# Outputs of one recurrence unit and scores of the next share one hook of an even step, half of the scores in the gate's bank

## The chip, the cores and the metric

The kernel runs on one core of a Trainium2 chip. The metric is the device time of one execution in microseconds (us); the time of a version is the median of its runs. Engines are called as in the profile: PE is TensorE, PEld its weight loads, DVE is VectorE, ACT is ScalarE, POOL is GpSimd, SP is SyncE, which issues most of the transfers.

## The reference

Three layers run one after the other: a linear-attention recurrence with decay (4 batches, 8 heads, 768 steps, head size 48), a dense gated layer (384 to 1536 and back, on 3072 tokens), and a mixture of 8 experts of which each token takes one.

```python
for t in range(S):                       # recurrence, per batch and head
    cur = einsum('bhd,bhe->bhde', u * k[t], v[t])
    y[t] = einsum('bhd,bhde->bhe', r[t], state + cur)
    state = w * state + einsum('bhd,bhe->bhde', k[t], v[t])
...
g = x @ w_gate                           # dense layer
x2 = (g * sigmoid(g) * (x @ w_val)) @ w_out
...
e_idx = argmax(x2 @ w_gate2)             # expert layer, one expert per token
out[mask] = gate_w * eom * (relu(x2[mask] @ w1[e]) @ w2[e])
```

## The kernel before

**Units.** The recurrence is cut into 6 chunks of 128 steps. A unit is one chunk of one batch (all 8 heads), so there are 24 units, `Unit(c, b)` with number `u.i = 4*c + b`. A unit has three pieces of work on PE: `scores(u)` (keys by receptances, L1615 and L1619), `outputs(u)` (the old state by receptances at L1646, then the masked scores by values at L1661 and L1672) and `state_terms(u)` (keys by values, L1689). Around them POOL scales keys and receptances by powers of the decay into `KW`, `RW` and `KH`; DVE sums the own terms (`sum_own`, L1107), masks the scores into `AM` (`mask_scores`, L1101, one instruction for each half of the scores, which stand in two PSUM banks), adds the state (`add_state`, L1132), the diagonals (`add_diagonals`, L1114) and the outputs into `X1` (`add_output`, L1124); ACT makes the diagonals (L793) and copies half of the outputs (`copy_output`). All matrices are single precision; the large products are split into high and low parts, three matmuls for one.

**Blocks and steps.** The dense layer runs in 6 blocks n of 512 tokens (one chunk of all 4 batches), each of 12 steps f, one for each 128 of the 1536 hidden values. In a step PE computes the gate (`up(GATE_PS, ...)`, 9 matmuls of 512 columns, L1734) and the value (`up(VALUE_PS, ...)`, 9 more), then, if there is one, a hook of recurrence work, then `down(n, f-1)` (9 matmuls, L1782 to L1784), the output product of the step before. The gate stands in bank 0, the value in bank 1, the outputs of the block in banks 2 to 4. ACT applies Silu to the gate (L868) and copies the high part (`AH`); DVE multiplies by the value (`PP`, L1325) and makes the low part (`AL`, L1328). Block n carries the 4 units of chunk n+1 in hooks of the steps 0 to 7; block 5 carries none. The order on every engine is written out by hand, and semaphores join them.

**Order of the hooks.** At an even step f PE does `state_terms` of the unit before and `scores` of unit f/2; at the odd step after it `outputs` of the same unit. The scores and the outputs of a unit share banks 5 and 6, so `scores(u)` waits until DVE has added the outputs of the unit before (`y_added`). Step 0 of a block from the second on has `turn` and `route_logits` (transposes and router logits of the block before) ahead of the hook, and the steps 9 and 10 have two small pieces of the router.

**First block.** Here the dense weights are also split. `STG` receives a piece of weights for two steps (six such pieces), ACT copies the high part (`WH`, three instructions), and DVE subtracts to get the low part (`WL`, `dense_lows`, L1142, three instructions of a third each, behind its hook work of an even step). PE waits for all three thirds of a piece (`dense_low`) before the gate of that piece's first step, and so ahead of steps 1, 2, 4, 6, 8 and 10:

```python
if first and (f == 1 or (f and f % 2 == 0)):
    pe.wait_ge(dense_low, 3 * (f // 2) + 3)
need(pe, silu_ready, q)
up(GATE_PS, 0, f, n).then_inc(gate_ready, 1)
need(pe, value_free, q)
...
up(VALUE_PS, 1, f, n).then_inc(value_ready, 1)
```

After the dense layer come 19 tiles of the expert layer, whose code the change does not touch.

Of the kernel before, what the change touches and what calls it, by code (L numbers as in the profile page):

```python
# [118 lines left out]
def rwkv_moe_moe(nc, unit_rk, unit_v, consts, w_dense, w_route, w1, w2, out):  # L119
# [89 lines left out]
    RW = place(a, "RW", [PR, PAIRS * P])  # L209
    KH = place(a, "KH", [P, PAIRS * PR])  # L210
# [80 lines left out]
    class Unit:  # L291
# [4 lines left out]
        def __init__(self, c, b):  # L296
# [21 lines left out]
            self.out = slice(b * P, b * P + P)  # L318

# [9 lines left out]
    def unit_before(u):  # L329
        return Unit(u.c, u.b - 1) if u.b else Unit(u.c - 1, BATCH - 1)  # L330
# [10 lines left out]
    with ctx:  # L341
# [139 lines left out]
        def _(sp):  # L481
# [8 lines left out]
            def load_two_ahead(u):  # L490
# [143 lines left out]
        def _(pool):  # L634
# [32 lines left out]
            def scale_r(u):  # L667
# [4 lines left out]
                else:  # L672
                    pool.wait_ge(y_ready, u.behind)
# [87 lines left out]
        def _(act):  # L761
# [18 lines left out]
            def first_state(b):  # L780
                u = Unit(0, b)
                act.wait_ge(u_ready, b // 2 * 2 + 2)
                for s in range(PAIRS):
                    last = nc.scalar.activation(ST[:, b, s, :], u.u[0:PR, s * VW:s * VW + VW], ACT.Copy, scale=WPOW[:, s, 7:8])
# [70 lines left out]
            def dense_block(n):  # L855
                first = isinstance(n, int) and n == 0
                last = isinstance(n, int) and n == CH - 1
                units = [] if last else units_of_block(n)
# [5 lines left out]
                for f in range(FT):  # L864
# [19 lines left out]
                    if f // 2 < len(units):  # L884
                        if f % 2 == 0:
                            diagonals(units[f // 2])
                        else:
                            copy_output(units[f // 2], n)
# [110 lines left out]
            with act.Fori(1, CH - 1) as n:  # L999
                dense_block(n)  # L1000
            dense_block(CH - 1)
# [27 lines left out]
        def _(dve):  # L1029
# [97 lines left out]
            def add_state(u):  # L1127
                dve.wait_ge(u_ready, u.i + 1)
                dve.wait_ge(state_ready, u.i - BATCH + 1)
                for s in range(PAIRS):  # L1130
                    used = Head(s).used
                    last = stt(out=ST[:, u.b, s, used], in0=ST[:, u.b, s, used], scalar=WPOW[:, s, 7:8],  # L1132
                               in1=u.u[0:PR, s * VW + used.start:s * VW + used.stop], op0=ALU.mult, op1=ALU.add)
# [175 lines left out]
            def dense_block(n):  # L1309
                first = isinstance(n, int) and n == 0  # L1310
                last = isinstance(n, int) and n == CH - 1
                units = [] if last else units_of_block(n)
# [3 lines left out]
                for f in range(FT):  # L1316
# [37 lines left out]
                    if f // 2 < len(units):  # L1354
                        u = units[f // 2]
                        if f % 2 == 0:
                            sum_own(u)
# [214 lines left out]
        def _(pe):  # L1572
# [288 lines left out]
            def dense_block(n):  # L1861
# [3 lines left out]
                for f in range(FT):  # L1865
# [6 lines left out]
                    if f == 1 and not first:  # L1872
                        pe.wait_ge(logits_copied, n)
# [187 lines left out]
```

## Time and profile before

| what | before |
|---|---|
| median of 3 runs | 836.19 us (835.34 to 836.27) |
| profiled execution, its time | 837.2 us |
| profiled execution, its span | 835.4 us |
| PE busy | 818.8 us, 98% |
| DVE, ACT, POOL busy | 485.8, 368.5, 201.2 us |
| granted PE clock | 0.999 of full speed |

PE is busy nearly the whole span, but its matmuls are pipelined and overlap in the record: a matmul of 512 columns is shown as 0.39 us long and the next one starts 0.23 us after it. So the busy share says little, and the distance from one start to the next is what is read here. In a timeline row the first number is the start in us from the span's start, the second the length of the group of equal instructions; a small matmul in full precision is recorded twice, so 16 of them stand as x32.

### The profile page before, as it was taken

How to read it: one execution, taken by the hardware profiler on the slowest of the kernel's cores; microseconds unless marked ns; L12 is line 12 of the kernel's file. 1: busy time of each engine (PE TensorE's matmuls, PEld its weight loads, DVE VectorE, ACT ScalarE, POOL GpSimd, SP SyncE). 2: the span in 40 equal slices, each digit the busy share in tenths (PEclk: the TensorE clock that was granted, in tenths of full speed). 3: DMA queues.
4: the chain of work that ended last, by engine and by line, in shares of the span. 5: the costliest groups of instructions: out<-in, count | busy, mean ns of one | idle time of the engine just before them, and what ended most of it. 6: DMA issues, size and time to landing. Idle time of an engine off the chain costs nothing.

```text
span 835.4 us, 19888 instructions
## 1 busy us (share of the span) xinstructions
PE 818.8 (98%) x7813; PEld 718.3 (86%) x7813; DVE 485.8 (58%) x1004; ACT 368.5 (44%) x705; POOL 201.2 (24%) x159
## 2 busy tenths in 40 slices
PE   7999999999999999999999999999999999999996
PEld 4777788888888888888888888899999999999996
DVE  7767635335543454435343453469968877897771
ACT  3644334223332143324332322456566776687661
POOL 3434204432354043502420210004021111111010
PEclk9999999999999999999999999999999999999999
DMA  8455203111221022302200116057997668766700
GB/s 336 159 170 170 70 4 119 62 60 40 88 96 61 10 90 85 98 1 97 87 1 2 39 39 260 6 223 230 336 389 261 244 252 294 294 251 242 285 18 19
DMA packets 24146, 116.72 MB, mean 140 GB/s; under 512 B 3372, under 2 KB 9824, under 8 KB 18448
## 3 DMA queue, kind: packets, MB, share of 16 engines
q1 hardware_dynamic: 19984, 101.16, 34.1%
q0 software_dynamic: 3520, 9.87, 3.1%
q10 hardware_dynamic: 576, 4.72, 1.6%
q8 instruction: 52, 0.85, 0.4%
q14 instruction: 14, 0.11, 0.0%
HBM read 102.64 MB, written 14.16 MB: 140 GB/s over the span
## 4 chain that ended last, share of the span: by engine, by line
PE 86%; DVE 7%; ACT 1%; issue 1%; DMA 1%; POOLq 0%; DVEq 0%; ACTq 0%
PE bank L1734 33%; PE bank L1782 6%; PE bank L1784 5%; PE bank L1783 5%; PE bank L1857 5%; PE bank L1855 5%; PE bank L1856 4%; PE bank L1816 3%; PE bank L1821 3%; PE bank L1822 3%; PE bank L1820 3%; DVE WL L1142 2%; PE bank L1661 1%; PE bank L1817 1%; PE bank L1615 1%
## 5 line engine op out<-in xcount | busy, mean ns | idle before, releaser
L1734 PE MATMUL bank<-X1H,WH 128*128 128x512 f32 x432 | 169.1, 392 | 2.6 <-DVE WL L1142 2.6
L1734 PE MATMUL bank<-X1L,WH 128*128 128x512 f32 x432 | 168.0, 390 | 0.2 <-DVE X1L L1148 0.2
L1734 PE MATMUL bank<-X1H,WL 128*128 128x512 f32 x432 | 168.0, 390 | 0.0
L1325 DVE TENSOR_TENSOR PP<-SG,bank 128x512 f32<-128x512 f32 (+1 forms) x78 | 49.8, 645 | 200.4 <-PE bank L1734 184.6
L763 ACT ACTIVATE AH<-PP 128x512 fp32r<-128x512 f32 (+1 forms) x78 | 46.0, 597 | 167.7 <-DVE PP L1325 167.7
L868 ACT ACTIVATE SG<-bank 128x512 f32<-128x512 f32 x72 | 43.0, 597 | 138.5 <-PE bank L1734 138.5
L1734 PEld LDWEIGHTS bank<-X1H,WH 128*128 128x128 f32 x432 | 81.0, 188 | 21.3 <-DVE WL L1142 4.3
L1734 PEld LDWEIGHTS bank<-X1H,WL 128*128 128x128 f32 x432 | 81.0, 188 | 17.3 <-DVE WL L1142 0.3
L1734 PEld LDWEIGHTS bank<-X1L,WH 128*128 128x128 f32 x432 | 81.1, 188 | 16.9 <-DVE X1L L1148 0.6
L1782 PE MATMUL bank<-AH,WH 128*128 128x512 f32 (+1 forms) x234 | 92.1, 394 | 0.0
L746 POOL DMA_INDIRECT out<-YO,IDX x31 | 38.7, 1248 | 218.1 <-ACT YO L962 208.9
L1784 PE MATMUL bank<-AH,WL 128*128 128x512 f32 (+1 forms) x234 | 87.7, 375 | 0.0
L1783 PE MATMUL bank<-AL,WH 128*128 128x512 f32 (+1 forms) x234 | 87.5, 374 | 0.0
L1328 DVE TENSOR_TENSOR AL<-PP,AH 128x512 fp32r<-128x512 f32 (+1 forms) x78 | 54.0, 699 | 51.2 <-ACT AH L763 51.2
L725 POOL DMA_INDIRECT store<-RC,POSI x24 | 26.0, 1084 | 199.0 <-DVE POSI L1240 171.4
L1782 PEld LDWEIGHTS bank<-AH,WH 128*128 128x128 f32 x234 | 44.0, 188 | 10.9
L793 ACT ACTIVATE DIAG<-CST,OWN_SUM 128x64 f32<-128x64 f32 x160 | 40.5, 336 | 29.2 <-DVE OWN_SUM L1107 27.7
L1822 PE MATMUL bank<-XH,W1L_ODD 128*128 128x256 f32 x189 | 52.2, 276 | 0.0
L1820 PE MATMUL bank<-XH,W1H_ODD 128*128 128x256 f32 x189 | 52.2, 276 | 0.0
L1821 PE MATMUL bank<-XL,W1H_ODD 128*128 128x256 f32 x189 | 52.2, 276 | 0.0
L1784 PEld LDWEIGHTS bank<-AH,WL 128*128 128x128 f32 x234 | 44.1, 188 | 8.1
L1783 PEld LDWEIGHTS bank<-AL,WH 128*128 128x128 f32 x234 | 44.2, 189 | 6.6
(238 smaller groups left out, 1825.4 us busy)
## 6 DMA issues: line engine op xcount, KB each, us to landing
W_EVEN<-w SPq DMA_DIRECT2D x20, 1536.0 KB, 8.5
W_ODD<-w SPq DMA_DIRECT2D x18, 1536.0 KB, 8.4
RK_IN<-unit_rk SPq DMA_DIRECT2D x19, 736.0 KB, 5.4
V_IN<-unit_v SPq DMA_DIRECT2D x20, 480.0 KB, 3.7
STG<-w_dense ACTq DMA_DIRECT2D x4, 1152.0 KB, 5.2
XG_ODD<-store SPq DMA_DIRECT2D x9, 394.0 KB, 8.6
store<-PAD SPq DMA_DIRECT2D x8, 394.0 KB, 5.2
STG<-w_dense SPq DMA_DIRECT2D x2, 1152.0 KB, 9.3
```

The source lines that it names most:

```text
L763: return nc.scalar.activation(out_, in_, ACT.Copy)
L868: nc.scalar.activation(SG[:, :], GATE_PS[:, :], ACT.Silu).then_inc(silu_ready, 1)
L1325: return tt(PP[:, part], SG[:, part], VALUE_PS[:, part], ALU.mult)
L1328: return tt(AL[:, par, part], PP[:, part], AH[:, par, part], ALU.subtract)
L1734: last = mm(bank_[:, :], lhs[:, f, m, k * P:k * P + P], rhs[:, k, :], start=(x == 0), stop=(x == len(terms) - 1))
L1782: mm(O_PS[m][:, t], WH[:, f, 2, w], AH[:, par, t], start=(f == 0), stop=False)
L1783: mm(O_PS[m][:, t], WH[:, f, 2, w], AL[:, par, t], start=False, stop=False)
L1784: last = mm(O_PS[m][:, t], WL[:, f, 2, w], AH[:, par, t], start=False, stop=(f == FT - 1 and x == 1))
L1820: mm(to, wh[:, w[k]], XH[:, k, :], start=(k == 0), stop=False)
L1821: mm(to, wh[:, w[k]], XL[:, k, :], start=False, stop=False)
L1822: last = mm(to, wl[:, w[k]], XH[:, k, :], start=False, stop=(k == KT - 1))
L1855: mm(YO_PS[half][:, 0:DM], HH[:, f, tk], wh[:, w], start=(f == 0), stop=False)
```

## The change

`outputs` of a unit move from an odd step into the even step after it, between `state_terms` of that unit and `scores` of the next one. So a hook of steps 2, 4, 6 and 8 has state terms and outputs of the unit that ends and scores of the unit that begins; the odd steps and step 0 (but for the first block's) have no hook. The scores get banks of their own: one half in bank 0, which is the gate's, the other in bank 7. The state terms go to the free columns of banks 5 and 6. `RW` gets a second buffer. In the first block the wait for the low weights is cut up, and the lows of the second piece are spread over two steps.

```diff
-                self.kw, self.rw, self.kh, self.am = KW, RW, KH, AM_PARTS
-                self.scores = self.y = bank[5], bank[6]
-                self.u = bank[7][:, PAIRS * VW:2 * PAIRS * VW]
+                self.kw, self.rw, self.kh, self.am = KW, (RW, RW_ODD)[self.odd], KH, AM_PARTS
+                self.scores = bank[0], bank[7]
+                self.y = bank[5], bank[6]
...
+    def unit_begun(n, f):
+
+        final = isinstance(n, int) and n >= CH - 2
+        if f in (2, 4, 6) and not (final and n == CH - 1):
+            return units_of_block(n)[f // 2]
+        if f == 0 and isinstance(n, int) and n == 0:
+            return units_of_block(n)[0]
+        if f == 8 and not final:
+            return units_of_block(n + 1)[0]
+        return None
+
+    def unit_ended(n, f):
+
+        if f in (2, 4, 6, 8) and not (isinstance(n, int) and n == CH - 1):
+            return units_of_block(n)[f // 2 - 1]
+        return None
...
                 def v_free():
-                    if u.last:
-                        sp.wait_ge(y_ready, u.i + 1)
-                    else:
-                        sp.wait_ge(u_ready, u.i + 1)
+                    sp.wait_ge(y_ready, u.i + 1)
...
                 else:
-                    pool.wait_ge(y_ready, u.behind)
+                    pool.wait_ge(y_ready, u.i - 1)
...
+                    begun, ended = unit_begun(n, f), unit_ended(n, f)
+                    if begun:
+                        sum_own(begun)
+                        mask_scores(begun)
+                    if ended:
+                        add_output(ended)
+                        if not ended.last:
+                            add_state(ended)
+                    if begun:
+                        add_diagonals(begun)
                     if first:
-                        if f % 2 == 0 and f // 2 + 1 < PIECES:
+                        if f == 0:
+                            dense_lows(1, (0,))
+                        elif f == 1:
+                            dense_lows(1, (1, 2))
+                        elif f % 2 == 0 and f // 2 + 1 < PIECES:
                             dense_lows(f // 2 + 1)
...
-                    if first and (f == 1 or (f and f % 2 == 0)):
-                        pe.wait_ge(dense_low, 3 * (f // 2) + 3)
+                    if first and f:
+                        pe.wait_ge(dense_low, 3 * (f // 2) + (2 if f % 2 else 1))
                     need(pe, silu_ready, q)
+                    if scores_of:
+                        pe.wait_ge(parts_masked, 2 * (scores_of.i - BATCH) + 1)
                     up(GATE_PS, 0, f, n).then_inc(gate_ready, 1)
...
+                    begun, ended = unit_begun(n, f), unit_ended(n, f)
+                    if ended:
+                        if not ended.last:
+                            state_terms(ended)
+                        outputs(ended)
+                    if begun:
+                        pe.wait_ge(silu_ready, q + 1)
+                        if f == 2:
+                            need(pe, ranks_copied, max(n - 1, 0))
+                        scores(begun)
+                    scores_of = begun
```

The rows below are the program's own order, each with the semaphores that its first instruction waits for. On PE, before, the hook of step 2 of the first block (state terms of the first carried unit, L1689, and scores of the next, L1615 and L1619) between the value and `down`:

```order
L1734 MATMUL bank<-X1H,WH 128x512 [waits value_free]
...
L1689 MATMUL bank<-V_IN_109,KH 32x48 [waits kt_scaled,state_ready]
...
L1615 MATMUL bank<-RW,KW 64x128 [waits y_added,k_scaled,r_scaled]
...
L1619 MATMUL bank<-RW,KW 64x64 x4
L1782 MATMUL bank<-AH,WH 128x512 [waits act_low]
...
L1734 MATMUL bank<-X1H,WH 128x512 [waits silu_ready]
```

On PE, with the change, the same place (state terms are L1714, outputs L1668, L1683 and L1694, scores L1636 and L1640, the gate and the value L1759, `down` from L1807):

```order
L1759 MATMUL bank<-X1H,WH 128x512 [waits value_free]
...
L1714 MATMUL bank<-V_IN_108,KH 32x48 [waits kh_copied,y_added,kt_scaled,state_ready]
...
L1668 MATMUL bank<-RW,ST 32x128 [waits parts_zeroed,state_ready,masked,y_added]
L1668 MATMUL bank<-RW,ST 32x128 x15
L1683 MATMUL bank<-AM,V_IN_108 32x128 [waits v_loaded0]
...
L1694 MATMUL bank<-AM,V_IN_108 32x64 x3
L1636 MATMUL bank<-RW_ODD,KW 64x128 [waits masked,r_scaled,silu_ready,k_scaled]
...
L1640 MATMUL bank<-RW_ODD,KW 64x64 x4
L1807 MATMUL bank<-AH,WH 128x512 [waits act_low]
...
L1759 MATMUL bank<-X1H,WH 128x512 [waits parts_masked,silu_ready,dense_low]
```

The outputs now stand between state terms and scores, and the gate of the next step waits for the mask as well. On DVE, before, an even and the following odd step of the first block:

```order
L1107 TENSOR_REDUCE OWN_SUM<-OWN 128x4 [waits diag_made,own_weighted]
...
L1101 TENSOR_TENSOR AM<-bank,CST 128x2x192 [waits scores_ready,causal_loaded,y_ready]
L1101 TENSOR_TENSOR AM<-bank,CST 128x2x192 [waits scores_ready]
L1132 SCALAR_TENSOR_TENSOR ST<-ST,WPOW,bank 112x48 [waits state_ready,u_ready]
...
L1114 TENSOR_TENSOR AM<-AM,DIAG 128x4x128 [waits parts_masked,diag_made]
L1142 TENSOR_TENSOR WL<-STG,WH 128x768 [waits dense_high] x3
L1325 TENSOR_TENSOR PP<-SG,bank 128x512 [waits act_low,value_ready,silu_ready]
L1328 TENSOR_TENSOR AL<-PP,AH 128x512 [waits act_high]
L1124 TENSOR_TENSOR X_118<-bank,X_118 128x3x128 [waits half_added,y_ready]
```

On DVE, with the change, the same two steps (masks L1119, outputs added L1142, state L1151, diagonals L1132, low weights L1161, `PP` L1343):

```order
L1119 TENSOR_TENSOR AM<-bank,CST 128x2x192 [waits scores_ready,causal_loaded,y_ready]
L1119 TENSOR_TENSOR AM<-bank,CST 128x2x192 [waits scores_ready]
L1142 TENSOR_TENSOR X_119<-bank,X_119 128x3x128 [waits half_added,y_ready]
L1151 SCALAR_TENSOR_TENSOR ST<-ST,WPOW,bank 112x48 [waits state_ready,y_ready,u_ready]
...
L1132 TENSOR_TENSOR AM<-AM,DIAG 128x4x128 [waits parts_masked,diag_made]
L1161 TENSOR_TENSOR WL<-STG,WH 128x768 [waits dense_high] x3
L1343 TENSOR_TENSOR PP<-SG,bank 128x512 [waits act_low,value_ready,silu_ready]
L1346 TENSOR_TENSOR AL<-PP,AH 128x512 [waits act_high]
```

The outputs are added in the even step, behind the masks and ahead of the low weights, and the odd step is left with `PP` and `AL`.

## Rows read from the trace of the kernel before

**Rows 1.** The page: busy time by engine.

```profile
PE 818.8 (98%) x7813; PEld 718.3 (86%) x7813; DVE 485.8 (58%) x1004; ACT 368.5 (44%) x705; POOL 201.2 (24%) x159
```

**Rows 2.** Waits of PE: what it sat idle for, total us, times, longest.

```profile
PE bank L1734 <- DVE WL L1142: 2.6, 4, 0.9
```

**Rows 3.** Timeline of PE, two gates of plain steps (block 1, steps 8 and 9).

```profile
179.36 0.39 PE L1734 MATMUL bank<-X1H,WH 128*128 128x512 f32 x1
185.48 0.39 PE L1734 MATMUL bank<-X1H,WH 128*128 128x512 f32 x1
```

**Rows 4.** Timeline of PE, an even hook (block 1, step 4).

```profile
152.16 0.39 PE L1734 MATMUL bank<-X1H,WL 128*128 128x512 f32 x1
152.48 0.54 PE L1689 MATMUL bank<-V_IN,KH 128*32 128x48 f32 x32
152.95 0.45 PE L1615 MATMUL bank<-RW,KW 48*64 48x128 f32 x8
...
153.78 0.50 PE L1782 MATMUL bank<-AH,WH 128*128 128x512 f32 x1
154.11 0.39 PE L1783 MATMUL bank<-AL,WH 128*128 128x512 f32 x1
```

**Rows 5.** Timeline of PE, an odd hook (block 1, step 3).

```profile
144.29 0.39 PE L1734 MATMUL bank<-X1H,WL 128*128 128x512 f32 x1
144.61 0.67 PE L1646 MATMUL bank<-RW,ST 48*32 48x128 f32 x32
...
145.94 0.27 PE L1661 MATMUL bank<-AM,V_IN 64*32 64x128 f32 x1
146.13 0.50 PE L1782 MATMUL bank<-AH,WH 128*128 128x512 f32 x1
146.47 0.39 PE L1783 MATMUL bank<-AL,WH 128*128 128x512 f32 x1
```

**Rows 6.** Timeline of PE, router logits to the last value matmul, block 2 and block 5.

```profile
211.89 0.86 PE L1752 MATMUL bank<-X2T,WROUTE 128*32 128x128 f32 x24
...
217.84 0.39 PE L1734 MATMUL bank<-X1H,WL 128*128 128x512 f32 x1
...
477.63 0.86 PE L1752 MATMUL bank<-X2T,WROUTE 128*32 128x128 f32 x24
...
482.41 0.39 PE L1734 MATMUL bank<-X1H,WL 128*128 128x512 f32 x1
```

**Rows 7.** Timeline of PE, first block, end of step 1 and gate of step 2.

```profile
39.99 0.39 PE L1784 MATMUL bank<-AH,WL 128*128 128x512 f32 x1
41.09 0.50 PE L1734 MATMUL bank<-X1H,WH 128*128 128x512 f32 x1 [0.71 <-DVE WL L1142]
```

**Rows 8.** Timeline of DVE, the even step of rows 4.

```profile
152.64 0.69 DVE L1325 TENSOR_TENSOR PP<-SG,bank 128x512 f32<-128x512 f32 x1 [5.15 <-PE bank L1734]
...
154.76 0.60 DVE L1107 TENSOR_REDUCE OWN_SUM<-OWN 128x4 f32<-128x192 f32 x2
155.28 1.01 DVE L1101 TENSOR_TENSOR AM<-bank,CST 128x384 f32<-128x384 f32 x2
```

**Rows 9.** Timelines of PE and DVE, first block, step 0 into step 1.

```profile
32.22 0.50 PE L1734 MATMUL bank<-X1H,WH 128*128 128x512 f32 x1
...
32.68 1.01 DVE L1101 TENSOR_TENSOR AM<-bank,CST 128x384 f32<-128x384 f32 x2
```

**Rows 10.** Timeline of DVE, first block, steps 2 and 3.

```profile
45.56 0.69 DVE L1325 TENSOR_TENSOR PP<-SG,bank 128x512 f32<-128x512 f32 x1 [2.07 <-PE bank L1734]
...
51.92 5.83 DVE L1142 TENSOR_TENSOR WL<-STG,WH 128x768 fp32r<-128x768 f32 x3
57.67 0.67 DVE L1325 TENSOR_TENSOR PP<-SG,bank 128x512 f32<-128x512 f32 x1
```

**Rows 11.** Timeline of POOL, first block: scaling of a unit's keys and receptances.

```profile
50.30 1.15 POOL L651 TENSOR_TENSOR OWN<-RK_IN,V_IN 128x448 f32<-128x448 f32 x1 [3.08 <-DMA V_IN<-unit_v]
...
54.93 2.00 POOL L674 TENSOR_TENSOR RW<-RK_IN,POWR 112x512 f32<-112x512 f32 x1
```

More of the change, by code:

```diff
@@ L318, in __init__, with u_slot @@
             self.out = slice(b * P, b * P + P)
+        def u_slot(self, s):
+            if self.first:
+                return self.u[:, s * VW:s * VW + VW]
+            return bank[5 + s // 2][:, DM + s % 2 * VW:DM + s % 2 * VW + VW]
         def wait_rk(self, engine):
@@ L883, in dense_block @@
                     copy(AH[:, f % 2, part], PP[:, part]).then_inc(act_high, 1)
[L884 to L888, printed above, removed]
+                    begun, ended = unit_begun(n, f), unit_ended(n, f)
+                    if ended:
+                        copy_output(ended, n)
+                    if begun:
+                        diagonals(begun)
                     if f == 0 and not first:
@@ L1595, in scores @@
                 else:
-                    pe.wait_ge(y_added, u.i)
-                    if isinstance(u.i, int) and u.i == BATCH:
-                        pe.wait_ge(state_ready, 2)
-                        pe.wait_ge(kh_copied, BATCH)
+                    if u.i == BATCH:
+                        pe.wait_ge(c_used, BATCH)
+                    else:
+                        pe.wait_ge(masked, 2 * u.i)
                     pe.nop(nofuse=True)
@@ L1873, in dense_block @@
                         pe.wait_ge(logits_copied, n)
+                    if first and f % 2:
+                        pe.wait_ge(dense_low, 3 * (f // 2) + 3)
                     up(VALUE_PS, 1, f, n).then_inc(value_ready, 1)
@@ L1881, in dense_block @@
                         if f == (1 if last else 9):
-                            pe.wait_ge(state_ready, UNITS - BATCH if last or units[-1].last else units[-1].i)
+                            if scores_of:
+                                pe.wait_ge(parts_masked, 2 * (scores_of.i - BATCH) + 2)
                             turn_logits(n)
@@ L1888, in dense_block @@
                         state_terms(u2)
-                    if f // 2 < len(units):
-                        u = units[f // 2]
-                        if f % 2 == 0:
-                            if f == 0 and not first:
-                                need(pe, ranks_copied, n - 1)
-                            if not (first and f == 0) and not unit_before(u).last:
-                                state_terms(unit_before(u))
-                            if first and f == 0:
-                                state_terms(u3)
-                            scores(u)
-                        else:
-                            outputs(u)
+                        state_terms(u3)
+                    begun, ended = unit_begun(n, f), unit_ended(n, f)
+                    if ended:
+                        if not ended.last:
+                            state_terms(ended)
+                        outputs(ended)
+                    if begun:
+                        pe.wait_ge(silu_ready, q + 1)
[3 more added lines that the diff above has]
+                    scores_of = begun
                     if f == 1:
```

34 lines of the change are left out of this document (13 added, 21 removed).

## The prediction

> **What bounds the kernel now.** I read the page first. PE is busy for 98% of the span, and the other engines stay at or below 58% [rows 1]. The waits of PE come next. In the dense part there is only one kind of any size, the low weights of the first block: four waits, 2.6 us together [rows 2]. So the dense layer is bound by the stream of matmuls itself, and the question becomes what the stream loses where nothing waits. For that I went to the timeline of PE and took differences between starts. A plain step, from one gate to the next, is 185.48 - 179.36 = 6.12 us for 27 matmuls [rows 3], which is 0.227 us a matmul.
>
> Against this a hook has a price. Even hook: from the last value matmul to the second `down` matmul are 154.11 - 152.16 = 1.95 us, of which two spacings (0.45) would be there anyway, so it costs **1.50** [rows 4]. Odd hook: 146.47 - 144.29 = 2.18, less 0.45, is **1.73** [rows 5]. Both have a way in (0.32 us to the first small matmul where 0.23 is plain: 0.09) and a way out. The reader is to see the way out in rows 5: 0.19 us from the last small matmul to the first `down`, and 0.34 instead of 0.23 to the second one, 0.30 together beyond the spacing. State terms and scores at step 0, which stand behind the router's logits, are cheaper, since they share a way in and out. From the logits to the last value matmul are 217.84 - 211.89 = 5.95 us with them, 482.41 - 477.63 = 4.78 in block 5, which has none: **1.17** [rows 6].
>
> **The merged hook.** No matmul is removed; the numbers of small matmuls are the same. What changes is the count of ways in and out. Price of a merged hook: way in 0.09, state terms 152.95 - 152.48 = 0.47 [rows 4], outputs to their last start 145.94 - 144.61 = 1.33 [rows 5], then an unknown x from the last output matmul to the first score, then scores with the way out, 154.11 - 152.95 - 0.23 = 0.93 [rows 4]. That is 2.82 + x. No row shows outputs followed by scores. From below, x is a spacing inside the group, 1.33 us over some 96 records, under 0.02. From above, it is the way from outputs to `down`, 0.19, or, if the scores have to wait until the last output matmul has ended, its shown length of 0.27 and some 0.05 of start, 0.32 [rows 5]. I take x = 0.17, near the way to `down`, because there too the shape changes from 64*32 tiles to another. The hook is then **2.99**, against 3.23 for the two that it replaces.
>
> The Trainium skill bears on x: its page TensorEngine Tiling (Array Packing), section Key Properties, says that a change of the tiling mode drains TensorE. Outputs (64*32) to scores (48*64) would be such a change, so the page speaks against the low end. With x = 0.02 the hooks would give 6.1 us, with the drain (0.19) 2.9. The gaps of 0.32 and 0.19 us beside a change of shape in rows 4 and 5 agree with it; no run here shows this pair.
>
> The sum over the blocks. Blocks 1 to 3 had 4 odd hooks (6.92), 3 even ones (4.50) and one at step 0 (1.17), 12.59 us each. Now they have 4 merged ones, 11.96. That saves 0.63 each, 1.9 together. Block 4 had the same but for the state terms of its even hooks (0.47 less each, 1.03), together 6.92 + 3.09 + 1.17 = 11.18. Now it has 3 merged hooks without state terms (2.52 each) and one of outputs alone (1.73), 9.29: 1.9 saved. Block 0 had 6.92 + 4.50 = 11.42 (its step 0 stays) and gets 11.96, since a pair of state terms and scores comes back from block 1: 0.5 lost. Together **3.2 us** saved. There are 19 merged hooks with outputs ahead of scores, so x moves this by 19 times its error: 6.1 us at x = 0.02, 0.4 us at x = 0.32.
>
> **The first block's waits.** The gate of step 2 starts 1.10 us after the last `down` matmul where 0.23 is plain: 0.87 lost, while the profile calls 0.71 of it idle [rows 7]. So each of the four waits costs 0.16 more than shown, 2.6 + 0.6 = 3.2 us, and the gate's first matmul is 0.50 long instead of 0.39, 0.11 more each: **3.7 us**. With the change the gate needs only the first third. At step 2 the first third starts as soon as ACT's high part is there, and `PP` of step 1 no longer stands behind all three. At steps 4, 6 and 8 the three thirds take 5.83 us on DVE [rows 10], so the first is ready some 3.9 us earlier than all. These waits go.
>
> What is late next is `PP` of the odd step. It stands behind the low weights on DVE, and the value matmuls two steps later wait until it has freed bank 1. From `PP` of the even step to the end of the following one are 57.67 + 0.67 - 45.56 = 12.78 us [rows 10]. DVE's hook work grows by `add_output`, about 0.5 us, most of which falls into the time in which DVE waits for ACT's diagonals, so I expect 12.9 to 13.4. The value of step f+2 wants bank 1 after the hook and its `down` (0.23 + 2.99 + 2.04), a plain step (6.12) and a gate (2.04), 13.4 us from the last value matmul, which is 0.48 us ahead of `PP` [rows 4, 8]: 12.9. That makes 0 to 0.5 us at each of the steps 4, 6, 8 and 10. I take **0.5 us** in all.
>
> A new wait stands at step 0 of the first block. It has no `down` behind its hook, and the gate of step 1 now needs the first half of the mask. That mask starts at 32.68 and takes 0.51 of the 1.01 for two, so the gate starts at about 33.25 instead of 32.22 [rows 9]: **1.0 us** lost.
>
> **What I cost at nothing.** The gate after a merged hook waits for the mask. Counted from the last value matmul, DVE is free for it after 155.28 - 152.16 = 3.12 us [rows 4, 8]; `down` starts after 0.32 + 0.47 + 1.33 + 0.17 + 0.83 = 3.12 and the last score ends about a tenth later, so the first half is masked by about 3.8 to 3.9, and the gate comes after 0.23 + 2.99 + 2.04 = 5.26. `down` covers it with 1.4 us to spare; without cover it would be 1.0 us a hook, as at step 0. The scores also wait for Silu of the gate whose bank they take; Silu is done before the value is. On POOL, receptances no longer wait for the outputs of the unit before, thanks to the second `RW`, so it has less to wait for. SP issues the load of `V_IN` after the outputs, about 1.3 us later in the hook than after the state terms. Queued behind that wait are the next loads of keys, and POOL waits for the values with the own products; from there to the end of `RW` are 56.93 - 50.30 = 6.6 us [rows 11], and a period of two steps is 15.2 us, so a late start has 3 to 5 us of room. The odd steps lose ACT and DVE work and have room. The expert part is not touched; it begins earlier by what is saved.
>
> **Sum.** -3.2 - 3.7 + 0.5 + 1.0 = -5.4 us. The profiled execution took 837.2 (span 835.4), 1.0 above the median of the runs; against its own time the sum gives 831.8. Against the median of 836.2 I predict **830.8 us**.
>
> **Rivals.**
> 1. *The odd step's `PP` takes over the wait of the low weights.* For it: POOL and DVE slow each other, three low parts took 5.83 us while POOL ran from 50.30 to 56.93 [rows 10, 11], and DVE has more ahead of them now. Against it: the value comes 2.04 us after the gate, and a merged hook is in between. It would cost about 0.5 us more at each of four steps, 2 us: 832.8. The Trainium skill (SBUF — State Buffer, Who interferes with whom) has it that a DVE instruction with two SBUF inputs and a GpSimd instruction exclude each other for their whole length. Rows 10 and 11 agree with it, and it would hold here.
> 2. *Merging saves nothing on PE.* If the small matmuls drain fully at each change of shape (x = 0.32), the hooks give 0.4 us and only the first block's 2.2 us are left: 833.6. Together with rival 1, 835.6, no change that can be measured (within 0.2%, 1.7 us, which is about what a measurement of this kernel can tell).
> 3. *The mask decides: slower.* Half of the scores sits in the gate's bank, so the whole stream of PE stands if DVE is late. In 19 hooks, 18 with `down` as cover, it costs whatever the mask is later than 5.2 us after the last value matmul. It decides from the point where the mask is 1.7 us later than I expect: each hook then waits 0.3 us and the 5.4 are gone. At 2.1 us late it is 0.7 us a hook, 12.6 us: 843. For it: DVE's two-input work is stretched by POOL, to about double in rows 10. Against it: at this place of an even step POOL has one short operation.
>
> **How the numbers follow.** Forecast (829 to 832.2): 0.62. Rival 1 alone: 0.12. Rival 2 alone: 0.07. x nearer to a plain spacing, 828 to 829: 0.05. Both of 1 and 2, or another wait of that size: 0.06. Rival 3, or a late load of values that does the same: 0.08. All but the last two are faster by over 0.2% (below 834.5): 0.86; same 0.06, slower 0.08. The range from 828.0 to 834.4 leaves out the two ends on the slow side and what lies under 828.
>
> **What the changed profile would show.** Hooks right: in block 1, from the last value matmul to the second `down` matmul of an even step, 3.4 us, and 6.12 us for odd steps. x right: 0.17 us between the last output matmul and the first score. First block right: no wait of the gate for `WL`, one wait of about 0.7 to 1.0 us on the mask `AM` at step 1, and waits on `PP` of under 0.5 us. The mask, if it is no bound, starts some 3.3 us after the last value matmul and PE waits for it nowhere else. Wrong would be a wait of PE for `AM` in every block, or hooks of 3.7 us.

## The result, and the profile after

| | before | after |
|---|---|---|
| median of the runs, us | 836.37 (835.16 to 837.61, 20 runs) | 837.74 (836.90 to 841.71, 20 runs) |
| profiled execution: time, span, us | 837.2, 835.4 | 838.89, 837.1 |
| granted clock, mean | 0.999 | 0.994 |

The ratio is 1.0019, 95% interval 1.0013 to 1.0025: some 1.5 us slower, on the edge of what a measurement of this kernel can tell from no change. The forecast was 830.8 (828.0 to 834.4).

The page's row of busy times is nearly that of before [rows 1]:

```profile
PE 818.0 (98%) x7813; PEld 722.2 (86%) x7813; DVE 482.0 (58%) x1004; ACT 369.2 (44%) x705; POOL 191.7 (23%) x159
```

The waits of PE (us in total, times, longest) first speak for the forecast. The low weights are gone from the list [rows 2], and the mask stands there once:

```profile
PE bank L1640 <- issue: 4.1, 2, 3.3
PE bank L1759 <- DVE AM L1119: 1.1, 1, 1.1
PE bank L1759 <- DVE X1L L1167: 0.2, 1, 0.2
```

The first of these waits is new. "issue" means that PE waited for nothing that the profile shows, and L1640 is the second kind of score matmul. Before looking there, a merged hook of block 1, in the timeline of PE (start, duration), with DVE's mask of the same step behind it:

```profile
154.32 0.39 PE L1759 MATMUL bank<-X1H,WL 128*128 128x512 f32 x1
154.63 0.54 PE L1714 MATMUL bank<-V_IN,KH 128*32 128x48 f32 x32
...
156.43 0.27 PE L1683 MATMUL bank<-AM,V_IN 64*32 64x128 f32 x1
156.63 0.45 PE L1636 MATMUL bank<-RW,KW 48*64 48x128 f32 x8
...
157.46 0.50 PE L1807 MATMUL bank<-AH,WH 128*128 128x512 f32 x1
157.79 0.39 PE L1808 MATMUL bank<-AL,WH 128*128 128x512 f32 x1
157.56 1.02 DVE L1119 TENSOR_TENSOR AM<-bank,CST 128x384 f32<-128x384 f32 x2
```

From the last value matmul to the second `down` matmul are 157.79 - 154.32 = 3.47 us (forecast 3.4), x is 156.63 - 156.43 = 0.20 (forecast 0.17), and the mask starts 3.24 us after the last value matmul (forecast 3.3). From gate to gate of their step 0, blocks 1 to 3 take 88.5 to 88.6 us where they took 89.1, and block 4 takes 85.8 where it took 87.6.

The whole miss stands in the first block. The gate of block 1 begins here at

```profile
122.57 0.40 PE L1759 MATMUL bank<-X1H,WH 128*128 128x512 f32 x1
```

and began at 117.25 before: 5.3 us later, where 1.7 earlier was forecast. The row of before:

```profile
117.25 0.40 PE L1734 MATMUL bank<-X1H,WH 128*128 128x512 f32 x1
```

The timeline of PE in the hook of step 2 shows why (in brackets: idle time before, and its end):

```profile
46.42 0.40 PE L1636 MATMUL bank<-RW_ODD,KW 48*64 48x128 f32 x8
46.65 0.22 PE L1640 MATMUL bank<-RW_ODD,KW 48*64 48x64 f32 x1
50.21 0.49 PE L1640 MATMUL bank<-RW_ODD,KW 48*64 48x64 f32 x7 [3.35 <-issue]
50.63 0.79 PE L1807 MATMUL bank<-AH,WH 128*128 128x512 f32 x1
51.22 0.63 PE L1808 MATMUL bank<-AL,WH 128*128 128x512 f32 x1
```

One score matmul of a group of eight runs, and the other seven start **3.56 us** later. There is no semaphore between them. The `down` matmuls behind the one at 51.22 are 0.43 us apart instead of 0.23. The windows (length, busy time of each engine, granted clock, share and rate of the DMA) say that this is the clock:

```profile
44.00:48.00 4.00, 2.86 (x154) 2.41 (x153) 1.90 (x4) 2.35 (x7) 1.15 (x1) 1.00 0.92 312
48.00:52.00 4.00, 1.79 (x10) 1.46 (x11) 1.18 (x3) 3.37 (x8) 0.84 (x1) 0.60 0.78 298
48.80:55.60 6.80, 5.39 (x19) 4.21 (x20) 4.78 (x9) 2.57 (x5) 4.44 (x4) 0.50 0.36 147
56.00:60.00 4.00, 4.00 (x19) 3.30 (x18) 3.30 (x3) 0.60 (x1) 1.08 (x1) 1.00 0.00 0
```

From 48.8 to 55.6 us the lower of the two levels was granted, 1.2 GHz, after PE had stood since 46.9. Some 11 spacings of 0.43 instead of 0.23 are about 2.3 us lost. A second gap of the same kind stands in the hook of step 8:

```profile
98.28 0.22 PE L1640 MATMUL bank<-RW,KW 48*64 48x64 f32 x1
99.28 0.28 PE L1640 MATMUL bank<-RW,KW 48*64 48x64 f32 x4 [0.79 <-issue]
```

3.56 + 2.3 + 1.0 = 6.9 us, against a miss of 5.3 + 1.7 = 7.0 at the gate of block 1. This is the profiled execution, which took 1.2 us more than the median. Its granted clock was 0.994; in 16 of the 20 launches it was 0.996, as in the trace of experiment 1 (in effect the same program), which has a stretch of 3.4 us at the lower clock and no gap at step 8. There the first block takes 95.8 us from its gate to that of block 1, and here 97.6.

What ends such a gap is seen only in the view of the DMA. It has one packet of 16 KB in queue q8, "instruction", at 47.97 to 48.95 us. A load of dense weights was issued 43.29 by ACT, and its packets (q10) fill the 16 DMA engines until 48.3. Here are the issue, then the queues from 44.3 to 47.9, then from 47.9 to 49 (packets, MB, share of the 16 engines):

```profile
STG<-w_dense ACTq DMA_DIRECT2D x1, 1152.0 KB, 5.3
...
q10 hardware_dynamic: 134, 1.17, 94.7%
q1 hardware_dynamic: 8, 0.03, 4.1%
...
q8 instruction: 1, 0.02, 5.6%
```

In the kernel before there is an instruction packet at 46.83 us, and PE doesn't stand. I also counted TensorE's records in the trace, weight loads and matmuls and semaphores, from its first one. The gaps stand right behind records 1473 and 2753. Both numbers are 193 more than a multiple of 256. A merged hook has 320 records of small matmuls in 3 us; the hooks that it replaces had 128 and 192.

### The profile page after: what moved, and what is told of

It is laid out like the page before. It is cut to its first block, busy times and chain, and to the rows that moved or that the text cites. A ratio compares the mean times of both kernels' runs of the same rounds, so it can differ in the third digit from the quotient of the medians.

```text
span 837.1 us, 19895 instructions
## 1 busy us (share of the span) xinstructions
PE 818.0 (98%) x7813; PEld 722.2 (86%) x7813; DVE 482.0 (58%) x1004; ACT 369.2 (44%) x705; POOL 191.7 (23%) x159
## 4 chain that ended last, share of the span: by engine, by line
PE 95%; issue 1%; POOLq 0%; DVE 0%; ACT 0%
PE bank L1759 35%; PE bank L1807 7%; PE bank L1808 6%; PE bank L1809 6%; PE bank L1880 5%; PE bank L1882 5%; PE bank L1881 5%; PE bank L1845 3%; PE bank L1846 3%; PE bank L1847 3%; PE bank L1841 3%; PE bank L1683 2%; PE bank L1668 1%; PE bank L1636 1%; PE bank L1821 1%; PE bank L1842 1%
## 5 line engine op out<-in xcount | busy, mean ns | idle before, releaser
L1343 DVE TENSOR_TENSOR PP<-SG,bank 128x512 f32<-128x512 f32 (+1 forms) x78 | 49.9, 646 | 211.1 <-PE bank L1759 186.5
L1759 PE MATMUL bank<-X1H,WH 128*128 128x512 f32 x432 | 168.9, 392 | 1.2 <-DVE AM L1119 1.1
L1759 PE MATMUL bank<-X1L,WH 128*128 128x512 f32 x432 | 168.3, 390 | 0.2 <-DVE X1L L1167 0.2
L1759 PE MATMUL bank<-X1H,WL 128*128 128x512 f32 x432 | 168.2, 390 | 0.0
L1759 PEld LDWEIGHTS bank<-X1H,WH 128*128 128x128 f32 x432 | 81.3, 188 | 19.1 <-issue 2.5
L1759 PEld LDWEIGHTS bank<-X1H,WL 128*128 128x128 f32 x432 | 81.2, 188 | 17.2 <-DVE WL L1161 0.3
L1759 PEld LDWEIGHTS bank<-X1L,WH 128*128 128x128 f32 x432 | 81.2, 188 | 17.1 <-DVE X1L L1167 0.7
L1807 PE MATMUL bank<-AH,WH 128*128 128x512 f32 (+1 forms) x234 | 91.4, 391 | 0.0
L1346 DVE TENSOR_TENSOR AL<-PP,AH 128x512 fp32r<-128x512 f32 (+1 forms) x78 | 55.6, 719 | 51.5 <-ACT AH L781 51.5
L1807 PEld LDWEIGHTS bank<-AH,WH 128*128 128x128 f32 x234 | 44.5, 190 | 9.0
L1880 PE MATMUL bank<-W2H_ODD,HH 128*128 128x384 f32 x144 | 49.0, 340 | 0.0
```

The source lines that it names most:

```text
L1343: return tt(PP[:, part], SG[:, part], VALUE_PS[:, part], ALU.mult)
L1346: return tt(AL[:, par, part], PP[:, part], AH[:, par, part], ALU.subtract)
L1759: last = mm(bank_[:, :], lhs[:, f, m, k * P:k * P + P], rhs[:, k, :], start=(x == 0), stop=(x == len(terms) - 1))
L1807: mm(O_PS[m][:, t], WH[:, f, 2, w], AH[:, par, t], start=(f == 0), stop=False)
L1880: mm(YO_PS[half][:, 0:DM], HH[:, f, tk], wh[:, w], start=(f == 0), stop=False)
```

## Experiments

Two theories. **A:** the gap is the stream of instructions. PE's program comes in pieces of 256 instructions, the next piece is asked for when a border is passed, and in a merged hook the 256 are used up before it is there, the more so when its transfer stands behind a load. **B:** the gap belongs to the merged hook as such, or to something that it waits for and the profile hides. Each ratio is against the kernel before, timed beside the run.

**1. Empty instructions at the start.** To move the borders:

```
+            for _ in range(128):
+                pe.nop(nofuse=True)
             pe.wait_ge(consts_loaded, 16)
```

> The changed kernel with 128 empty instructions ahead of PE's first wait, where PE idles anyway. It shifts the places at which PE needs its next piece of code, and nothing else. Theory A (PE runs dry in the hooks of steps 2 and 8 of the first block because the transfer of its next code stands behind the 1152 KB load of weights): the gaps of 3.5 and 1.0 us inside the scores move to other places or go, and the time changes by 2 us or more, most likely to some 831 to 835. Theory B (a merged hook has too many instructions whatever else runs): the gaps stay in those hooks, within 1 us of the changed kernel. Theory C (a semaphore or an engine other than PE holds the scores): no change at all.

838.10 us (837.14 to 841.83), ratio 1.0021 (1.0011 to 1.0032). The gap was 3.63 us behind record 1473 again. The empty instructions left no record and moved nothing, so this is in effect a repeat of the changed kernel. It says that the gap comes back at the same place, and nothing on the theories. What did not come back is the gap at step 8, and the lower clock lasted 3.4 us instead of 6.8.

**2. A lighter load.** The loads of pieces 3 to 6 of the dense weights bring a sixth, 192 KB; the rest of these weights is left out.

```
-                act.dma_start(STG[:, :, :, :], w_dense[:, 2 * p:2 * p + 2, :, :]).then_inc(stage_loaded, 16)
+                act.dma_start(STG[:, 0:1, 0:1, :], w_dense[:, 2 * p:2 * p + 1, 0:1, :]).then_inc(stage_loaded, 16)
```

> The changed kernel with the loads of the third to sixth piece of dense weights cut to a sixth (192 KB); the rest of those weights is left out, all instructions stay. Theory A: with the large transfer gone, the transfer of code is not delayed, both gaps go, the clock stays at 2.4 GHz in the first block, about 7 us less than the changed kernel, 830.5 to 832. Theory B or C: gaps stay, 837 to 838. That weights were late would also be excluded or shown here: if it were so, waits on WL would be seen in the changed kernel, and none are.

833.49 us (832.78 to 838.75), ratio 0.9968 (0.9955 to 0.9982). Timeline of PE at the gap:

```profile
47.04 0.22 PE L1640 MATMUL bank<-RW_ODD,KW 48*64 48x64 f32 x1
48.23 0.34 PE L1640 MATMUL bank<-RW_ODD,KW 48*64 48x64 f32 x7 [0.97 <-issue]
```

The place is the same, record 1473, but the gap is 1.19 us instead of 3.56, and the clock doesn't fall behind it. The gap at step 8 is gone too, and a small one of 0.56 us stands behind record 3521. So most of the gap at step 2 is the load, and a third of it is there without, against what theory A had foretold: from the passing of record 1217 to the going on are 3.5 us here, and the 256 records pass in 2.35. (In the changed kernel it is 5.9 us.)

**3. The first hook's scores in banks 5 and 6**, so that step 1 doesn't wait for the mask:

```
-                self.scores = bank[0], bank[7]
+                self.of_first_hook = isinstance(c, int) and self.i == BATCH
+                self.scores = (bank[5], bank[6]) if self.of_first_hook else (bank[0], bank[7])
...
-                    if scores_of:
+                    if scores_of and not scores_of.of_first_hook:
```

> The changed kernel with the scores of the first carried unit alone (hook of step 0 of the first block) in banks 5 and 6, so that the gate of step 1 does not wait for the mask. My price of that wait was 1.0 us and the trace shows 1.1: so 1.1 us less than the changed kernel, about 836.6. If the wait only moves (PE then waits for the low weights at step 1), 0 to 0.5 us. The gaps inside the scores may change too, since everything after comes 1.1 us earlier while the load of weights hangs on DVE: by theory A the time may then fall or rise by some us, by B and C it may not.

838.18 us (836.80 to 839.33), ratio 1.0017 (1.0005 to 1.0029). Waits of PE:

```profile
PE bank L1643 <- issue: 4.3, 2, 3.9
PE bank L1762 <- ACT SG L886: 0.4, 1, 0.4
```

The wait for the mask is gone. But 0.4 us of it came back as a wait for Silu, and the first gap grew from 3.56 to 4.21: what was gained ahead of it was given back in it, and of the 1.1 us that were expected nothing shows in the median.

**4. The finer waits alone.** The kernel before, with the low weights waited for in thirds, and no merging:

```
-                    if first and (f == 1 or (f and f % 2 == 0)):
-                        pe.wait_ge(dense_low, 3 * (f // 2) + 3)
+                    if first and f:
+                        pe.wait_ge(dense_low, 3 * (f // 2) + (2 if f % 2 else 1))
...
+                    if first and f % 2:
+                        pe.wait_ge(dense_low, 3 * (f // 2) + 3)
```

> The kernel before with the finer wait for the low weights alone (gate of an even step waits for one third, gate and value of the odd one for two and three thirds). My price of the four waits was 3.7 us. If PP of the odd step, which stays behind all three thirds on DVE, does not take over, 832.7; since here the value comes 2.04 us after the gate and PP only 0.7 us after the low weights, 1.4 us of each wait can go, and the four were 0.33 to 1.04: so all of them, 832.5 to 833.5. By rival 1 of the prediction about half, 834.5.

833.93 us (832.40 to 838.32), ratio 0.9978 (0.9964 to 0.9993), span 831.2. There is no gap of over 0.3 us in its dense part, and the gate of block 1 stands at

```profile
113.57 0.40 PE L1734 MATMUL bank<-X1H,WH 128*128 128x512 f32 x1
```

against 117.25 before: 3.7 us, just the term of the prediction.

**5. Four more with empty instructions**, 64 or 96 of them, on the changed kernel and on those of 3 and 4. As in experiment 1 the empty instructions leave nothing in the trace, so these are repeats.

> The changed kernel with 64 empty instructions ahead of PE's first wait. With 128 of them the large gap stood at the same matmuls as without, which theory A explains only if code comes in pieces of 128 instructions (or a divisor). Theory A then: 64 move the edge of a piece by half a piece, out of the first part of the hook of step 2, so that the next piece is asked for before the load of weights starts at 44 us. The 3.6 us gap and the half clock behind it (2.3 us) go, 831 to 833. If pieces are 64 or fewer instructions, or by theory B (a merged hook always outruns its code), the gap stays, 837 to 838.

> The changed kernel with the first hook's scores in banks 5 and 6 (no wait for the mask at step 1) and the 64 empty instructions. By theory A the 1.1 us of the mask wait now count, less what the low weights and Silu keep of them (0.8 at step 2 in the run with the banks alone): 0.3 to 1.0 us below the run with 64 empty instructions alone. By theory B as the changed kernel.

> The changed kernel with 96 empty instructions. By theory A the gaps depend on where the edge of a piece falls, so the gap is at another place or of another size than with 0, 64 and 128; no number is forecast within 830 to 838, but its size and the time must go together, 1.6 us of time for each us of gap above 3 (as the clock follows) and 1 for 1 below. By theory B the gap is the same 3.6 us at the same matmuls.

> Control: the kernel before with the finer waits alone and 64 empty instructions. Its hooks are apart, and it has no gap without them. If empty instructions as such cost or gain nothing, it takes the same time as the finer waits alone, 833.9, within 0.7 us; theory A allows a small gap of up to 1 us, since the edges move here too.

The changed kernel: 837.68 and 838.33 us, gaps of 3.58 and 3.91 behind record 1473. That of 3: 838.49 us, gap 4.20. That of 4: 833.10 us (832.71 to 833.28), ratio 0.9952 (0.9934 to 0.9969), no gap.

So the changed program stands in four traces (the changed kernel, 1 and two of these). The gap at step 2 is in all of them, 3.56, 3.63, 3.58 and 3.91 us; the one behind record 2753 is 1.00, none, 0.58 and 0.35 us; and the lower clock lasted 6.8, 3.4, 3.4 and 6.8 us.

**6. Small matmuls at the start.** A matmul in full precision is four records (two weight loads, two matmuls), and these do stay in the program. 24 of them (96 records) stand behind the warm-up of the changed kernel and of those of 3 and 4, and 8 of them (32 records) in the changed kernel:

```
+            for x in range(24):          # or 8
+                mm(bank[2][:, 0:32], ident, CST[:, C_ID:C_ID + 32], start=True, stop=True)
```

> The empty instructions of the earlier runs left no record and shifted nothing, so real ones now: the changed kernel with 24 small matmuls (96 records on PE) behind the two warm-up matmuls, where PE idles until 9.4 us. In all versions the gaps stand right behind PE's records 1473, 2753 and 3521 counted from the start, which are 5 and 3 times 256 apart. Theory A (code comes in pieces of 256 records, asked for at a border, and the piece asked for during the load of weights arrives late): the border that fell into the hook of step 2 just as the load started now falls into the matmuls of step 1; the 3.6 us gap, the half clock behind it and the 1.0 us gap go, what is left are gaps of at most 0.6 us behind records 1473 + 256 k. 831 to 832.5. Theory B (merged hooks outrun their code wherever the border falls): a gap of over 2 us in the first block stays, 836 to 838.

> The shift of 96 together with the first hook's scores in banks 5 and 6. Theory A: as the shift of 96 alone, less what the mask wait costs net: 0.3 to 0.8 us less, 830.5 to 832.

> Control: the kernel before with the finer waits alone, and the same 24 small matmuls. Its hooks have at most 192 records, under a piece of 256, and it has no gap. If the small matmuls cost nothing themselves, 833.1 to 834 like the finer waits alone; a gap of up to 1 us may come by theory A. The difference from the shift of 96 in the changed kernel is then what merging the hooks is worth without gaps: 3.2 by my sum with x = 0.17, 2.6 with the x of 0.20 that the trace shows, less 1.1 for the mask: 1.5 to 2.

> The changed kernel with 8 small matmuls (32 records) at the same place. Theory A: the border falls 32 records earlier in the hook of step 2, still within it and still as the load starts. So the large gap stays, still behind record 1473, but 32 records earlier in the hook (in the third quarter of the scores or at their start), and is not smaller, 3.6 to 4.5 us; 837 to 839. If the gap belonged to a certain matmul or a wait, it would stand behind record 1505.

With 96 records: 842.96, 842.40 and 844.68 us, all far over what was expected. In the first of the three the windows show the clock:

```profile
8.00:12.00 4.00, 4.00 (x27) 3.03 (x25) 2.50 (x4) 0.88 (x4) 0.00 (x0) 1.00 1.02 405
12.00:24.00 12.00, 11.85 (x130) 11.01 (x133) 3.78 (x6) 1.64 (x3) 1.19 (x1) 0.57 0.50 204
```

The small matmuls (48 in the trace) run from 9.3 to 16.5 us. At 12.9 us, 3.6 us after they began, the granted clock went to its lower level, and the first block begins 8.7 us later than in the changed kernel. That is the cost of the matmuls and of the clock in this launch, and it hides what they moved. It is not the whole story of the medians: in each of the three kernels the launches with a granted clock of 0.997 or 0.998 (843.5 to 848.0 us) took longer than all those with 0.989 to 0.993 (840.4 to 844.7), and no trace shows what they lost. Yet the gap in the hook of step 2 was gone in both kernels with merged hooks. From the first block's gate to that of block 1 the first of them takes 124.14 - 33.72 = 90.4 us, the changed kernel 97.6, the kernel before 92.5. The comparison for which the finer waits alone got the same 24 matmuls came out: 842.96 is 1.7 us below 844.68 (1.5 to 2 expected), though with 6 and 5 launches the intervals of the ratios overlap.

With 32 records theory A as I had it foretold that the gap stays, since border 1473 still lies inside the hook. It was gone. The profiled span was 832.3. From 837.1, less 6.9 for what went, with 1.1 for the matmuls and 0.8 for a new gap behind record 8129 (31 x 256 + 193), it would be 832.1. So the place was right and my rule for when the piece is asked for was wrong: the instruction packet came at 42.30 us, ahead of the hook and of the load. Over the launches the gain did not hold: 836.62 us (834.07 to 841.52), ratio 1.0006 (0.9989 to 1.0023). The traced launch (834.17) was the second fastest of 12, and what the others lost is open.

**7. Small matmuls where PE waits anyway.** The last three runs put 4, 8 or 16 of them in front of the gate of step 1 in the first block, where PE waits 1.1 us for the mask, into the value bank, which is free then:

```
+                    if first and f == 1:
+                        pe.wait_ge(value_free, q)
+                        for x in range(4):          # or 8, or 16
+                            mm(VALUE_PS[:, 0:32], ident, CST[:, C_ID:C_ID + 32], start=True, stop=True)
                     if scores_of:
                         pe.wait_ge(parts_masked, 2 * (scores_of.i - BATCH) + 1)
```

> The changed kernel with 8 small matmuls (32 records, 1.06 us of TensorE in the run with 8 of them at the start) put into the 1.1 us in which TensorE waits for the mask ahead of the gate of step 1. They cost nothing there and move the borders of the 16 KB code transfers 32 records back, as in the run with 8 at the start, where the transfer began at 42.3 us, ahead of the 1152 KB load. Theory A (the miss is the code transfer queued behind the load, in the middle of a merged hook): both gaps of the first block and the half clock behind them go, span 837.1 - 3.6 - 2.3 - 1.0 = 830.2 us, up to 831.1 with the gap of 0.8 us that the run with 8 at the start had at 328 us; median 831.5 to 834. Theory B (the gap belongs to the merged hook of step 2 as such, whatever stands at the border): the gap stays at 3.6 us and the median at 837 to 838. Theory C (the small matmuls take from the mask wait nothing, they delay the gate): one microsecond more, 832.5 to 835.

> The same with 4 small matmuls (16 records). The border before then stands 38 records behind the start of the hook of step 2, between the 22 of the run with 8 (no gap) and the 54 of the changed kernel (3.6 us). Theory A with a fetch that is asked for some fixed number of records ahead of the border: if that number is over 38, no gap and 831.5 to 834, if it is under, the gap of 3.6 us behind the 1473rd record and 837 to 838. Theory B: 837 to 838.

> The same with 16 small matmuls (64 records, 2.1 us, of which 1.1 us lie in the wait). Theory A: no gap at step 2, since the border before lies ahead of the hook, and 1.0 us more than with 8: median 832.5 to 835. Theory B: 838 to 839.

**With 4 (16 records): 831.81 us (831.11 to 832.49), ratio 0.9946 (0.9928 to 0.9965), span 829.3.** Its timeline of PE shows the small matmuls, the scores of step 2, now in one piece, and the gate of block 1:

```profile
31.55 1.08 PE L1898 MATMUL bank<-CST 128*128 128x32 f32 x8
32.59 0.50 PE L1759 MATMUL bank<-X1H,WH 128*128 128x512 f32 x1
...
45.39 0.40 PE L1636 MATMUL bank<-RW_ODD,KW 48*64 48x128 f32 x8
45.61 0.29 PE L1640 MATMUL bank<-RW_ODD,KW 48*64 48x64 f32 x8
45.84 0.50 PE L1807 MATMUL bank<-AH,WH 128*128 128x512 f32 x1
...
114.67 0.40 PE L1759 MATMUL bank<-X1H,WH 128*128 128x512 f32 x1
```

The gate of step 1 comes no later than with the mask wait (1.04 us after the first small matmul; from the start of the last group of scores it is 1.27 us, against 1.36 in the changed kernel). There is no gap and no fall of the clock in the dense part. The view of the DMA from 42.2 to 43.4 us has the instruction packet at 42.29, while the load is only being issued:

```profile
q8 instruction: 1, 0.02, 4.8%
issues: line engine op xcount, KB each, median us to landing
STG<-w_dense ACTq DMA_DIRECT2D x1, 1152.0 KB, 5.3
```

With 8 (32 records): 833.78 us (833.31 to 838.72), ratio 0.9975 (0.9961 to 0.9989), no gap at step 2, but one of 1.17 us behind record 8129 (the traced launch took 836.18; its first block begins 1.9 us later than with 4). With 16 (64 records): 839.65 us (836.17 to 841.60), ratio 1.0035 (1.0021 to 1.0049), far from the 832.5 to 835 expected. The gap at step 2 is gone there too, but three others have come, behind records 1985, 4033 and 6081, of 1.12, 1.67 and 1.29 us, and 3.3 us of small matmuls are again followed by half clock (windows of the stretch of small matmuls and of one behind it):

```profile
31.90:35.20 3.30, 3.30 (x37) 3.30 (x30) 2.04 (x6) 2.67 (x12) 3.30 (x4) 1.00 0.59 191
36.30:39.70 3.40, 3.40 (x10) 2.68 (x9) 1.71 (x1) 2.62 (x4) 1.52 (x2) 0.51 0.00 0
```

What follows: the same merged hook at the same place, with the same load, stands 3.56 us or not at all, by 16 records of shift. Every gap of over 0.45 us within a merged hook of these kernels stands 193 records behind a multiple of 256. Theory B falls. Of theory A, the place is shown by the shifts and the part of the load by run 2. That the packet in q8 is what PE waits for is not named by any wait of the profile. It rests on its times (PE goes on 1.3 us after its end in the changed kernel) and on its pace: in the changed kernel the 50th packet begins when 12,745 records of PE have begun, which is one for each 255. (Behind it a loop of seven rounds repeats PE's instructions, and 2,826 records pass without a packet.)

When a piece is asked for stays partly open. The border one piece ahead (record 1217) is 54 records behind the first of the hook in the changed kernel, 38 and 22 with 16 and 32 records of shift. In the latter two the packet came before the load, in the first behind it. So PE's sequencer seems to look at least 38 and less than 54 records past the instruction on which it waits. The packets themselves narrow it: among the first 50 of every trace, none begins more than 43 records ahead of its border, and several begin 41 ahead.

## Why the prediction was wrong

**What held.** The merged hook: 3.47 us to the second `down` against 3.4, and x = 0.20 against 0.17. Blocks 1 to 3 gave 0.5 to 0.6 us each (forecast 0.63) and block 4 gave 1.8 (1.9). The waits for low weights: 3.7 us by run 4 (3.7). The mask at step 1: 1.06 us idle (1.0), by these rows of the changed kernel, PE's and DVE's:

```profile
33.63 0.47 PE L1759 MATMUL bank<-X1H,WH 128*128 128x512 f32 x1 [1.06 <-DVE AM L1119]
...
32.94 1.01 DVE L1119 TENSOR_TENSOR AM<-bank,CST 128x384 f32<-128x384 f32 x2
```

The waits for `PP` were forecast at 0.5 us and none came; that term was a little too dear, and rival 1 fell with it, though POOL does stretch DVE's work as it says: each of the three low parts of rows 10 takes 1.9 to 2.05 us beside POOL, where the first ones, at 25.7 us, take 0.95. The sum of -5.4 us can be tested on the last experiment with 4 small matmuls, which differs from the changed kernel by these matmuls and the border that they move: from the first block's gate to that of block 5 it takes 441.8 us where the kernel before takes 447.4, 5.6 less. Its span is 6.1 us under that of before, and its median, which is what the forecast was for, 4.3 us under the median of before in its session, 831.8 against a forecast of 830.8. Most of this is the finer waits: between the same two gates experiment 4 takes 443.7, so the merged hooks with their mask wait were worth 1.9 us.

**What failed** is the sentence with which the price of the merged hook begins: "No matmul is removed; the numbers of small matmuls are the same. What changes is the count of ways in and out." Something else changes too, how many instructions stand close together. The hooks before had 128 to 192 records and a run of long matmuls between them; the merged one has 320 in 3 us, and 256 of them pass in 2.3. In that time a piece of the program has to be fetched. In the changed kernel it took from the passing of record 1217 at 44.33 us to the going on at 50.21, and 3.6 us of this had passed before the packet began, while the load's packets filled the queues. The prediction had put this at nothing without a reason: it had no term for it, and no rival was about issue. In its place the runs showed 6.9 us in the first block of the profiled execution. Rival 3 had the right sign and the wrong mechanism: the mask is never late after step 1.

The second mistake is smaller. I gave 0.14 to all outcomes that are not faster, "same" and "slower" together, because all the waits that I looked for were those between engines. A row that spoke of it was there, in the waits of PE of the kernel before:

```profile
PE bank L1689 <- issue: 0.3, 1, 0.3
```

It ends at 23.75 us, behind record 705, which is 2 x 256 + 193.

The Trainium skill has the mechanism in its page Runtime: NRT & Kernel Launch, section Instruction fetch mechanics: the instruction memory is refilled in blocks of 16 KiB, 256 instructions, by the sequencer's own DMA queue, and the cost of passing a block is "mostly hidden". The size and the spacing agree with the traces here (packets of 16384 bytes, gaps at one remainder of 256). "Mostly hidden" holds for the kernel before and not for this one, where two crossings in the first block cost 6.9 us with what followed from the clock.

## What to carry to other kernels

Where a change packs many short TensorE instructions together, count them: some 256 within less time than a fetch takes can stall (here they pass in 2.3 us, and with the light load 3.5 us went by from the border to the going on, 2.4 of them from the packet's start), and if a large load is issued just ahead, the fetch stands behind it. Look for "issue" as the releaser within a group of like matmuls, and for the instruction packet in the view of the DMA. A few records more or less ahead of the place decide, so a change that is judged by one timing may be judged by where the borders happened to fall: move them by a dozen instructions, in a place where the engine waits anyway, before giving up the change.

## What the runs showed of the hardware

- In the changed kernel PE stood for 3.35 us from 46.9, and from 48.8 the granted clock was at its lower level for 6.8 us; in two of the three repeats with the empty instructions the stretch was 3.4 us. In the run with 16 small matmuls in the wait, 3.3 us of matmuls of 32 columns were followed by 3.4 us at the lower level; in the run with 24 at the start the level fell 3.6 us after they began and stayed for 10.2. Behind the stalls of 0.8 to 1.7 us it did not fall.
- PE's instructions arrive in packets of 16384 bytes, one for each 255 records or so. From a packet's start to the end of a stall behind it were 2.2 to 2.8 us.
- From the last 64*32 matmul to the first 48*64 one are 0.20 us from start to start, where plain spacing is under 0.02.
- Empty instructions (`nop`) without a wait leave no record on TensorE and shift no border. A full-precision matmul of 32 columns takes four records and 0.2 to 0.3 us.
- The same program, launched again, can keep, shrink or lose such a gap: the one behind record 2753 was 1.00, 0.58, 0.35 us or none in four traces.
